# Attention and a two-layer block on one core: the value product in two blocks instead of four, transposed units in a new order, one weight split moved to GpSimd

## The reference, cut

```python
# q, k, v: (4, 8, 576, 64); w_in: (512, 2048); w_out: (2048, 512); alpha: (2048,)
q_rot, k_rot = rotate(q), rotate(k)          # rotary embedding over position
scores = matmul(q_rot, k_rot^T) / sqrt(64)
attn = exp(scores - max(scores)); attn = attn / (sum(attn) + 1e-09)
x = (attn @ v).transpose(0, 2, 1, 3).reshape(4 * 576, 512)
h = x @ w_in
g = maximum(h, 0) + alpha * minimum(h, 0)
out = g @ w_out
```

## Time and profile before

| | |
|---|---|
| median of three runs | 752.54 us (749.11 to 753.39) |
| profiled execution: time | 750.56 us |
| profiled execution: span | 748.6 us |
| TensorE busy | 705.3 us, 4100 matmuls |
| VectorE, ScalarE, GpSimd busy | 398.0, 316.5, 250.0 us |
| granted TensorE clock | full (2.4 GHz level) in all 40 slices |
| attention, up to the first output product | 345 us |
| two-layer block behind it | 403 us |

### The profile page before, as it was taken

The page is one execution under the profiler, slowest core; times in us unless marked ns, Lnnn a source line. Parts: engine busy times, 40 slices in busy tenths (PEclk is TensorE's granted clock), DMA queues, the critical chain, the costliest instruction groups (busy, mean ns, idle before and its releaser), DMA issues.

```text
span 748.6 us, 12146 instructions
## 1 busy us (share of the span) xinstructions
PE 705.3 (94%) x4100; PEld 587.6 (78%) x4100; DVE 398.0 (53%) x696; ACT 316.5 (42%) x756; POOL 250.0 (33%) x234
## 2 busy tenths in 40 slices
PE   4789999999999999999999999999999999999996
PEld 3666676776776776776988999999999999999995
DVE  4656666677667777757998333323323333342321
ACT  2656666666666666642222322222232222223222
POOL 6355544445555454001322222222222222222221
PEclk9999999999999999999999999999999999999999
DMA  6765655555544554506000100000010001000001
GB/s 161 187 159 123 161 117 125 126 126 124 123 112 113 115 120 109 146 11 220 0 1 1 43 0 1 15 29 0 1 42 0 0 0 42 0 0 30 14 0 43
DMA packets 76619, 51.30 MB, mean 69 GB/s; under 512 B 61089, under 2 KB 61473, under 8 KB 76065
## 3 DMA queue, kind: packets, MB, share of 16 engines
q1 hardware_dynamic: 76576, 50.76, 27.2%
HBM read 22.95 MB, written 4.72 MB: 37 GB/s over the span
## 4 chain that ended last, share of the span: by engine, by line
PE 60%; issue 18%; DVE 7%; ACT 4%; POOL 4%; DMA 3%; SPq 3%; POOLq 0%; ACTq 0%; DVEq 0%
PE banks L569 17%; PE banks L597 17%; PE banks L513 8%; PE banks L535 8%; PE banks L484 7%; POOL g_lo L422 2%; DMA raw_k<-in_k 2%; PE banks L528 2%; PE banks L453 2%; ACT prob L644 2%; DVE pt L820 2%; ACT pt L684 1%; SPq L274 1%; DVE nmax L783 1%; SPq L291 1%
## 5 line engine op out<-in xcount | busy, mean ns | idle before, releaser
L422 POOL TENSOR_TENSOR g_lo<-g,g_hi 128x384 fp32r<-128x384 f32 x96 | 102.5, 1068 | 339.5 <-ACT g_hi L736 339.5
L891 DVE TENSOR_SCALAR g<-banks,alpha_sb 128x384 f32<-128x384 f32 x96 | 59.2, 617 | 226.7 <-ACT pos L728 226.7
L783 DVE TENSOR_REDUCE nmax<-banks 128x1 f32<-128x576 f32 x144 | 108.6, 754 | 63.6 <-PE banks L484 61.2
L569 PE MATMUL banks<-x_hi,w_in_hi 128*128 128x384 f32 x384 | 129.9, 338 | 0.0
L569 PE MATMUL banks<-x_lo,w_in_hi 128*128 128x384 f32 x384 | 128.9, 336 | 0.0
L569 PE MATMUL banks<-x_hi,w_in_lo 128*128 128x384 f32 x384 | 128.0, 333 | 0.0
L597 PE MATMUL banks<-w_out_hi,g_hi 128*128 128x512 f32 x288 | 113.7, 395 | 5.1 <-DVE w_out_lo L882 3.7
L728 ACT ACTIVATE pos<-banks 128x384 f32<-128x384 f32 x96 | 47.1, 491 | 167.2 <-PE banks L569 167.1
L597 PE MATMUL banks<-w_out_hi,g_lo 128*128 128x512 f32 x288 | 112.6, 391 | 0.0
L597 PE MATMUL banks<-w_out_lo,g_hi 128*128 128x512 f32 x288 | 112.1, 389 | 0.0
L736 ACT ACTIVATE g_hi<-g 128x384 fp32r<-128x384 f32 x96 | 50.5, 526 | 128.1 <-DVE g L894 128.1
(11 more groups left out here) (86 smaller groups left out, 910.2 us busy)
## 6 DMA issues: line engine op xcount, KB each, us to landing
k_two<-k_hi SPq DMA_DIRECT2D x64, 160.0 KB, 2.9
out<-stage SPq DMA_DIRECT2D x18, 256.0 KB, 2.0
raw_q<-in_q SPq DMA_DIRECT2D x32, 128.0 KB, 2.5
raw_k<-in_k SPq DMA_DIRECT2D x32, 128.0 KB, 2.8
q_two<-q_hi SPq DMA_DIRECT2D x32, 128.0 KB, 2.3
q_two<-q_lo SPq DMA_DIRECT2D x32, 128.0 KB, 2.3
q_own<-q_hi SPq DMA_DIRECT2D x32, 128.0 KB, 2.3
raw_v<-in_v SPq DMA_DIRECT2D x32, 128.0 KB, 2.4
```

The lines of the kernel that those rows point to most:

```text
L422: nc.gpsimd.tensor_tensor(g_lo[f % 2][:, :], g[f % 2][:, :], g_hi[f % 2][:, :].bitcast(F32), ALU.subtract).then_inc(g_lo_done, 1)
L569: mm = nc.tensor.matmul(h_ps[f % 2], w[:, j, cols], xx[:, j, :], start=(step == 0), stop=(step == 3 * CT - 1))
L783: nc.vector.tensor_reduce(nmax[:, t % 2, n:n + 1], s_ps[(t * TILES + n) % 2], AX.XY, ALU.max, negate=True).then_inc(max_done, 1)
L891: nc.vector.tensor_scalar(g[f % 2][:, :], h_ps[f % 2], 0.0, alpha_sb[:, f:f + 1], ALU.min, ALU.mult).then_inc(neg_done, 1)
```

## The change

- UNITS_IN and the unit numbers are new. The remainder-query units (U_QREM 0, U_KQREM 1) of a pair are transposed in the next period, ahead of its score 0 (UNITS_FIRST), and both are taken out by VectorE. Slot 0 has no other unit; slot 1 has KREM and two PB units, slot 2 the two others, slot 3 Q, slot 4 the inverses, slot 5 K and QKREM, slot 6 two PA units, slots 7 and 8 one each.
- The value product of a half is one block: half 0 in slot 3, half 1 in slot 7. Normalise is in slots 5 and 8.
- ScalarE takes out only the first of its units of a slot ahead of the exponential, the others behind it. The inverse remainder goes to VectorE.
- GpSimd splits w_in: three slabs in eight pieces of 256 columns in periods 4 to 11 (a rounding addition of zero behind k's rotation, a subtraction behind q's), the fourth slab in four pieces of 512 columns behind the last period. VectorE's `split_w_in` is gone.
- The SBUF map is new: w_in_hi has a place of its own beside the attention's tiles, q_two, q_own and k_two lie together, inv_wide lies on inv_sb. The w_out loads wait for the last score, not for value products. The splits of x for the first chunk are in slots 1, 3, 5 and 7 of period 15; they were in slot 4 of periods 12 to 15.

```diff
-U_KREM = 0
-U_PB = (1, 2, 3, 4)
-U_INV, U_INV_REM = 6, 7
-U_Q, U_K, U_QKREM = 5, 8, 11
-U_PA = (9, 10, 12, 13)
-U_QREM, U_KQREM = 14, 15
+U_QREM, U_KQREM = 0, 1
+U_KREM = 2
+U_PB = (3, 4, 5, 6)
+U_Q = 7
+U_INV, U_INV_REM = 8, 9
+U_K, U_QKREM = 10, 11
+U_PA = (12, 13, 14, 15)
 UNITS = 16
-OF_PREV = (U_KREM, *U_PB, U_INV, U_INV_REM)
+OF_PREV = (U_QREM, U_KQREM, U_KREM, *U_PB, U_INV, U_INV_REM)
 OF_NEXT = (U_Q, U_K, U_QKREM)
-BY_ACT = (U_KREM, U_PB[1], U_PB[3], U_INV, U_INV_REM, U_PA[1], U_PA[3], U_KQREM)
-BY_DVE = (U_PB[0], U_PB[2], U_PA[0], U_PA[2], U_QREM)
-
-
-UNITS_IN = ((0, 1), (2,), (3, 4), (5,), (6, 7), (8, 9), (10, 11), (12, 13), (14, 15))
+BY_ACT = (U_KREM, U_PB[1], U_PB[3], U_INV, U_PA[1], U_PA[3])
+BY_DVE = (U_QREM, U_KQREM, U_PB[0], U_PB[2], U_INV_REM, U_PA[0], U_PA[2])
+
+
+UNITS_FIRST = (U_QREM, U_KQREM)
+UNITS_IN = ((), (2, 3, 4), (5, 6), (7,), (8, 9), (10, 11), (12, 13), (14,), (15,))
 HIDDEN_IN = (0, 2)
-PV_IN = {3: (0, 0), 4: (0, 1), 5: (1, 0), 6: (1, 1)}
-NORMAL_IN = {6: 0, 7: 1}
+PV_IN = {3: 0, 7: 1}
+NORMAL_IN = {5: 0, 8: 1}
+X_IN = (1, 3, 5, 7)
...
+        w_in_hi = sb(ctx, "w_in_hi", [P, CT, F], F32R)
...
+            inv_wide = inv_sb[:, 0:QT * P].rearrange("p (i d) -> p i d", i=QT)
...
-                    sp.wait_ge(pv_done, 2 * PERIODS - 2)
-                    sp.wait_ge(turned, unit_count(PERIODS, U_PB[-1]))
-                elif f == FT // 2:
-                    sp.wait_ge(pv_done, 2 * PERIODS)
+                    sp.wait_ge(scored, PERIODS * TILES)
...
+            def high_w_in(slabs, first, count):
+
+                cols = bass.ds(first, count)
+                nc.gpsimd.tensor_tensor(w_in_hi[:, slabs, cols], w_in_raw[:, slabs, cols],
+                                        zero[:, :].unsqueeze(2).to_broadcast([P, slabs.stop - slabs.start, count]),
+                                        ALU.add).then_inc(w_in_high, 1)
+            def low_w_in(slabs, first, count):
+
+                cols = bass.ds(first, count)
+                nc.gpsimd.tensor_tensor(w_in_lo[:, slabs, cols], w_in_raw[:, slabs, cols],
+                                        w_in_hi[:, slabs, cols].bitcast(F32), ALU.subtract).then_inc(w_in_split, 1)
...
+                    n = p - PAIRS
+                    if not isinstance(b, int):
+
+                        pool.wait_ge(w_in_in, 16 * (CT - 1))
+                        high_w_in(slice(0, CT - 1), n * W_COLS, W_COLS)
+                        pool.wait_ge(w_in_high, n + 1)
                     if has_pair(p + 2):
                         rope(p + 2, 0)
+                    if not isinstance(b, int):
+                        low_w_in(slice(0, CT - 1), n * W_COLS, W_COLS)
 
             batches(pool, batch)
+            pool.wait_ge(w_in_in, 16 * CT)
+            for n in range(F // W_LAST):
+                high_w_in(slice(CT - 1, CT), n * W_LAST, W_LAST)
+                pool.wait_ge(w_in_high, 2 * PAIRS + n + 1)
+                low_w_in(slice(CT - 1, CT), n * W_LAST, W_LAST)
...
-            def pv(p, par, h, part):
+            def pv(p, par, h):
 
                 n = (p - 1) * 2 + h
                 cols = slice(h * HALF, (h + 1) * HALF)
-                if part == 0:
-                    if h == 0:
-                        pe.wait_ge(v_in, p * 64)
-                        for u in (U_QREM, U_KQREM):
-                            pe.wait_ge(evac[u % 2], evac_count(p - 1, u))
-                        pe.wait_ge(evac[U_KREM % 2], evac_count(p, U_KREM))
-                    if not (isinstance(n, int) and n < 2):
-                        pe.wait_ge(x_done, n - 1)
-                    nc.tensor.matmul(o_ps[h], raw_v[par][:, QT, :], pt[:, PT_REM, cols], start=True, stop=False)
                 if h == 0:
-                    for u in U_PB[2 * part:2 * part + 2]:
+                    pe.wait_ge(v_in, p * 64)
+                    for u in U_PB[2:]:
                         pe.wait_ge(evac[u % 2], evac_count(p, u))
-                for j in range(part * QT // 2, (part + 1) * QT // 2):
+                if not (isinstance(n, int) and n < 2):
+                    pe.wait_ge(x_done, n - 1)
+                nc.tensor.matmul(o_ps[h], raw_v[par][:, QT, :], pt[:, PT_REM, cols], start=True, stop=False)
+                for j in range(QT):
                     for head in range(2):
                         own = slice(head * D, (head + 1) * D)
                         mm = nc.tensor.matmul(o_ps[h][own, :], raw_v[par][:, j, own], pt[:, pt_slot(par, head, j), cols],
                                               start=False, stop=(j == QT - 1))
-                if part == 1:
-                    mm.then_inc(pv_done, 1)
+                mm.then_inc(pv_done, 1)
...
                 for slot in range(TILES):
+                    if slot == 0 and has_prev(p):
+                        for u in UNITS_FIRST:
+                            turn(p, t, u)
                     if has_now(p):
...
-                        pe.wait_ge(exp_done, PERIODS * TILES)
-                    pe.wait_ge(w_in_split, 2 * (f + 1))
+                        pe.wait_ge(exp_done, PERIODS * TILES - 1)
+                    pe.wait_ge(w_in_split, 2 * PAIRS + f // (FT // 4) + 1)
...
+                    of_act = [u for u in UNITS_IN[slot] if exists_now(p, u) and u not in BY_DVE]
+                    for u in of_act[:1]:
+                        hi(p, u, t) if u in OF_NEXT else flat(p, u, t)
                     if has_now(p):
                         exps(p, t, slot)
+                    for u in of_act[1:]:
+                        hi(p, u, t) if u in OF_NEXT else flat(p, u, t)
                     if slot == 4 and has_now(p):
...
-            def split_w_in(f):
-
-                cols = slice(f * P, (f + 1) * P)
-                if f == 0:
-                    dve.wait_ge(w_in_in, 16 * CT)
-                    dve.wait_ge(scored, PERIODS * TILES)
-                nc.vector.tensor_copy(w_in_hi[:, :, cols], w_in_raw[:, :, cols]).then_inc(w_in_split, 1)
-                dve.wait_ge(w_in_split, 2 * f + 1)
-                nc.vector.tensor_tensor(w_in_lo[:, :, cols], w_in_raw[:, :, cols], w_in_hi[:, :, cols].bitcast(F32),
-                                        ALU.subtract).then_inc(w_in_split, 1)
...
-                    if not has_now(p) and slot == TILES - 1:
-                        split_w_out(0)
                     if 1 <= slot <= 3 and has_prev(p):
                         reciprocals(p, t, slot - 1)
-                    if not has_now(p) and slot < len(HIDDEN_IN):
-                        split_w_in(slot)
                     for u in UNITS_IN[slot]:
                         if exists_now(p, u):
                             if u in OF_NEXT:
...
                                 flat(p, u, t)
                     if has_prev(p) and slot in NORMAL_IN:
                         normalise(b if t else b - 1, (t - 1) % PAIRS, p, NORMAL_IN[slot])
-                    if slot == 4 and isinstance(b, int) and b == NB - 1:
-                        split_x(0, 0, t)
+                    if not has_now(p) and slot == TILES - 1:
+                        split_w_out(0)
+                    if slot in X_IN and isinstance(p, int) and p == PERIODS - 1:
+                        split_x(0, 0, X_IN.index(slot))
                     if slot == 5 and not has_now(p):
                         dve.wait_ge(alpha_in, 16)
                         gate(0, 0, 0)
 
+            nc.vector.memset(zero[:, :], 0.0).then_inc(padded, 1)
             dve.wait_ge(padded, PADDED)
             dve.wait_ge(sin_in, 16)
```

More of the change, by code:

```diff
@@ L57, in build @@
     PERIODS = NB * PAIRS
-    PADDED = 14
+    PADDED = 15
+    W_COLS = F // (2 * PAIRS)
+    W_LAST = F // 4
     Q_STACKED, K_STACKED = 6 * 16, 4 * 16
@@ L147, in build @@
             q_lo = sb(att, "q_lo", [P, QT * P], F32R)
[L149 to L157, removed]
+            k_hi, k_lo, q_two, q_own, k_two = [], [], [], [], []
+            for i in range(2):
+                k_hi.append(sb(att, f"k_hi{i}", [P, REM + S], F32R))
+                k_lo.append(sb(att, f"k_lo{i}", [P, REM + S], F32R))
+                if i == 0:
+                    early = used[0]
+            for i in range(2):
+                q_two.append(sb(att, f"q_two{i}", [P, 2, QT * P], F32R))
+                q_own.append(sb(att, f"q_own{i}", [P, 2, QT * P], F32R))
+                k_two.append(sb(att, f"k_two{i}", [P, 2, REM + S], F32R))
+            of_scores = used[0]
+            raw_v = [sb(att, f"raw_v{i}", [P, ST, P]) for i in range(2)]
             qrem_hi = sb(att, "qrem_hi", [P, P], F32R)
             qrem_lo = sb(att, "qrem_lo", [P, P], F32R)
+            until_prob = used[0]
             prob = sb(att, "prob", [P, QT, 2 * S])
@@ L170, in build @@
             inv = sb(att, "inv", [P, 2, TILES])
-            inv_wide = sb(att, "inv_wide", [P, QT, P])
             ident = sb(att, "ident", [P, P])
-            kept = used[0]
-            q_two.append(sb(att, "q_two1", [P, 2, QT * P], F32R))
```

(16 more changed lines are left out.)

78 lines of the change are left out of this document (32 added, 46 removed).

## The result

The changed kernel takes 776.08 us (median of four, 775.36 to 776.35) against 751.02 for the kernel before, a ratio of 1.033 (95% interval 1.029 to 1.037): slower, inside the stated range, 4 us above the point. Its profiled execution took 775.36 us with a span of 773.6; before it was 750.56 and 748.6.

What follows compares the result with a forecast made beforehand. TensorE, busy 94% of the span, and holds of its in-order queue bound the kernel. +21.8 + 2.3 + 0.8 - 1.0 - 3.0 = +20.9 on 750.56 or 752.54 gave 772 us, range 757 to 785.

Steps and rivals of the forecast that it cites:

- The walk through the period: Periods 4 to 14: each engine's queue followed in time, 21.67 us a period against 19.69, +21.8 us in all.
- The price of the two blocks: Value product in two blocks: two entries and exits fewer, 0.48 us a period off TensorE.
- Periods 1 to 3: Early periods, lengthened before by late loads: 65.0 us against 62.74, +2.3 us.
- Step 3, the last period: Period 15 and the turn to the second part, until the first output: 33.7 us against 34.66, -1.0 us.
- The rule of the Trainium skill: Copy into inv_wide, periods 4 to 11: late by the rule, but 2 us of room, so nothing moves.
- Step 4, the first chunk: First chunk of the second part: w_in's split off VectorE gains 3.0 us, at worst 1.5.
- overlapping waits: Rival for the periods: early waits shrink later ones, +1 us a period, 757 to 761 us; chance 0.10.

## Why the prediction was right, and where it was not

**The walk through the period** held: 21.57 against 21.67, with six of the eight waits printed where they were put; K's 0.14 shows only in the starts (11.28 below), and the 0.17 ahead of score 6 did not come. In the walk's terms, at a remainder score of 204.32: PB1 at 3.35 (3.32), Q at 6.12 (6.13), K at 11.28 (11.22), PA0 at 13.35 (13.39), PA1 at 14.75 (14.86), PA2 at 16.38 (16.47), the next score at 21.66 (21.67). Every hand-over was taken from a row of the same kind of unit, and the order of each engine's queue was walked, not its load. Shown by experiment: the order carries the loss (put back: 19.67). With the exponential out of QKREM's chain 0.7 of it goes, with the cover back behind K and QKREM 1.8; these two are no sum, since the exponential costs something only where the cover is missing.

**The price of the two blocks.** The 0.48 saved on TensorE is consistent with the row of sixteen (2.09 between starts) but was never measured alone; the run with two blocks on the kernel before gives only the net, 0.48 the other way, in which older waits shrank too.

**Periods 1 to 3** came out 0.9 better than said: outside the loop a period takes 21.3, and the walk had been set up from rows of a period inside it.

**Step 3, the last period, failed.** -1.0 was forecast, +1.2 came: 1.35 of the difference up to the next remainder-query transposes (19.18 for 17.83), 0.87 behind them (16.72 for 15.85). The step has no term for the x splits, which the change moves into period 15. VectorE, GpSimd and TensorE, changed kernel:

```profile
345.12 1.23 POOL L402 TENSOR_TENSOR w_in_hi<-w_in_raw,zero 128x512 fp32r<-128x512 f32 x1
345.49 1.28 DVE L885 TENSOR_TENSOR x_lo<-x,x_hi 128x384 fp32r<-128x384 f32 x1
...
366.93 0.99 POOL L457 TENSOR_TENSOR g_lo<-g,g_hi 128x384 fp32r<-128x384 f32 x1 [16.70 <-ACT g_hi L750]
367.08 1.13 DVE L891 CAST w_out_hi<-w_out_raw 128x512 fp32r<-128x512 f32 x1
```

```profile
348.08 0.66 PE L548 MATMUL banks<-ident,prob 128*128 128x128 f32 x4 [1.18 <-DVE pt L838]
...
369.04 0.47 PE L629 MATMUL banks<-w_out_hi,g_hi 128*128 128x512 f32 x1 [2.39 <-DVE w_out_lo L893]
```

The x split's subtraction, which starts beside GpSimd's last slab, takes 1.28 for 0.56; PA0's copy is late by it, and PA2 waits 1.18 in the first of TensorE's rows. With this x split in slot 7, in the changed kernel with the w_out split ahead, the stretch took 1.1 less.

w_out's first cast takes 1.13 for 0.42, since it starts just after g_lo has started on GpSimd, and the wait ahead of the first output product grew from 1.67 to 2.39. This is not the moved w_in split but the moved normalise: in slot 5 it stands ahead of the gate of step 0, so that the gate and g_lo come later, and g_lo then meets w_out's split. All kernels here whose first normalise stands in slot 5 wait 2.38 or 2.39 there, the one with two blocks on the old map and without any w_in work on GpSimd too; the three that have it in slot 6 wait 1.66 or 1.67. The two terms make 1.8 of the 2.2; the rest was not traced.

The rule of the Trainium skill that the prediction weighed ("GPSIMD Engine Reference", "Key points": GpSimd shares its SBUF interfaces with VectorE) was judged for the copy of the inverses in the periods in the loop, where GpSimd's split of three slabs indeed costs nothing (21.68 a period without it). It was not carried to period 15 nor, as the next step shows, to the first chunk.

**Step 4, the first chunk, failed.** -3.0 was forecast, nothing came. The prediction took VectorE's work for the limit, 1.63 a step removed against 0.76 missing, with -1.5 as the least that would come. The chain of the changed kernel in that stretch:

```profile
398.44 0.50 ACT pos L742
...
398.96 0.63 DVE g L902
...
400.48 0.56 DVE x_lo L885
401.04 1.17 DVE w_out_hi L891
...
403.07 2.29 PE banks L629 x9
```

From the end of the hidden product at 398.42 to the output product at 403.07 there is a chain: ScalarE's positive part, the gate, the x split, both halves of the w_out split. w_in's split stood behind w_out's in VectorE's order and was not in it. The reading of the earlier trace rows had one member of this chain and the busy time, and not its order. The run with the w_out split ahead shows what was needed.

The same stretch holds something else. The w_out cast of a step without an x split, and g_lo on GpSimd in the step with one:

```profile
395.93 0.42 DVE L891 CAST w_out_hi<-w_out_raw 128x512 fp32r<-128x512 f32 x1
```

```profile
400.81 1.11 POOL L457 TENSOR_TENSOR g_lo<-g,g_hi 128x384 fp32r<-128x384 f32 x1 [2.86 <-ACT g_hi L750]
```

The x split pushes the cast behind the start of g_lo, and beside it the cast takes 1.25 for 0.42. These 0.8 us are more than the 0.51 that TensorE waits, and the 1.17 in the earlier trace rows was such a stretched cast already. So it is an estimate from these rows, which no run isolates, that without the meeting of VectorE and GpSimd the x split would have fitted in. In the run with the w_out split ahead the cast is as long (1.24) but no longer in the chain.

**A term that was missing.** From the first output product to the end 1.2 us more. Output products in the chain of the changed kernel, 43 steps apart, and of the kernel before, 37 apart:

```profile
451.27 2.08 PE banks L629 x9
...
630.15 2.08 PE banks L629 x9
```

```profile
452.22 2.06 PE banks L597 x9
...
605.65 2.06 PE banks L597 x9
```

It is 4.160 a step against 4.147; 90 steps make 1.2. TensorE's code in the loop is the same. Every kernel here with the new map has 4.16, also the one with the old order, and the three on the old map have 4.147. So it goes with the map, or with GpSimd's work on w_in, which the same eight kernels have but which is long done in these steps; the map alone, or one tile's place, was not tried.

**Forecast and hit.** Of the +25.0, 20.9 were forecast; the two failed steps and the missing term are 6.4, and the inner and early periods give 2.3 back. The range held because the loss per period, 20.7 of the 25.0, was right; the misses of steps 3 and 4 were allowed for in its width.

**A rival's sum.** For overlapping waits the prediction adds 14 - 4 + 2, which is 12 and puts the time at 763 to 765, not at the 757 to 761 written beside it. So that rival lay inside the forecast, and its 757 to 761 lies inside the range that is said to leave half of it out. The forecast and its range are made up of other terms.

## What to carry to other kernels

Where transposed units alternate between two banks, a bank's turnaround (here 1.35 us for a plain unit, 2.0 to 2.9 for one with a high and a low part) has to be covered by TensorE work that stands between the two fills; long products are that cover, and merging them was only worth it here where the merged block stood behind the slowest turnaround. Walk the queue of each evacuating engine: its load did not show any of these waits. Taking work off an engine pays only if that work was in the chain; where two things hold one place, each edit alone can measure as nothing. And a duration in a row may itself be the fault: compare it with the shortest of its line, and look at what GpSimd does beside it.

## What the runs showed of the hardware that was not expected

- A VectorE copy from SBUF to SBUF (0.42 us) that met two GpSimd memsets of 5.23 us each took 8.26 us and ended 0.3 us after the second: it waited for a whole instruction and then for the next one behind it. Beside GpSimd instructions of 1.0 to 1.5 us an x split's cast took 1.1 to 1.4 for 0.35, its subtraction 1.3 to 1.5 for 0.56, and a w_out cast 1.13 to 1.25 for 0.42. VectorE's maximum and copies out of PSUM kept their times (0.74 to 0.76 and 0.67 to 0.69) beside the same GpSimd work in period 15 of the changed kernel. This agrees in kind with the rule above; how long the wait is went with the length of GpSimd's instructions.
- A step of 21 matmuls is 0.013 us (0.3%) longer in all eight kernels with the new map; whether the places of the tiles are the reason was not tested alone.
